# Seven block products for eight in the gated stage of an attention, mixture-of-experts and gated-product kernel

## The reference, cut to what matters

```python
x = attention(q, k, v)          # sink of 4 keys, window of 128
for e in range(8):              # each token goes to one expert, 192 tokens an expert
    h = np.maximum(x[mask_e] @ w1[e], 0.0)
    y[mask_e] = h @ w2[e]
a = y @ w_a                     # (1536 x 512) @ (512 x 1536)
b = y @ w_b
out = (a * b) @ w_out           # (1536 x 1536) @ (1536 x 512)
```

## Time and profile before

| | us |
|---|---|
| median of 3 runs | 674.89 |
| the runs | 673.66 to 678.23 |
| the profiled execution, its own time | 676.53 |
| its span, first to last instruction | 674.8 |
| PE busy | 627.0 (93%) |
| DVE, ACT, POOL busy | 319.2, 312.7, 138.9 |

### The profile page before, as it was taken

One profiled execution on the slowest core, in us unless ns is written; L12 is line 12 of the kernel. 1 busy time (PEld: TensorE's weight loads), 2 busy tenths in 40 slices (PEclk: granted clock), 3 DMA queues, 4 the chain that ended last, 5 costly groups with the idle time before them and its releaser, 6 DMA issues.

```text
span 674.8 us, 10427 instructions
## 1 busy us (share of the span) xinstructions
PE 627.0 (93%) x3696; PEld 527.9 (78%) x3696; DVE 319.2 (47%) x904; ACT 312.7 (46%) x720; POOL 138.9 (21%) x83
## 2 busy tenths in 40 slices
PE   7999999999443999999999999999999999999995
PEld 4877766776322999999999888888888887888784
DVE  3677665772674577877777321213222222222221
ACT  3576655762230577777777241415141415141411
POOL 4000000000004222112222023223431414340502
PEclk8998999999555999999999999999999999999999
DMA  9964150230403356666675314131523232432001
GB/s 187 268 141 95 48 169 28 67 107 16 134 0 92 98 199 239 214 224 223 216 244 180 131 46 141 59 130 62 186 65 122 72 114 86 163 106 80 0 0 62
DMA packets 85813, 81.25 MB, mean 120 GB/s; under 512 B 39696, under 2 KB 62224, under 8 KB 85776
## 3 DMA queue, kind: packets, MB, share of 16 engines
q1 hardware_dynamic: 83856, 74.49, 36.5%
q0 software_dynamic: 1920, 6.29, 2.8%
HBM read 74.48 MB, written 6.29 MB: 120 GB/s over the span
## 4 chain that ended last, share of the span: by engine, by line
PE 87%; DVE 5%; ACT 3%; issue 2%; DMA 1%; POOL 1%; DVEq 0%; ACTq 0%; POOLq 0%
PE psum L1478 15%; PE psum L1471 15%; PE psum L1472 14%; PE psum L1473 14%; PE psum L1479 7%; PE psum L1291 5%; PE psum L1269 3%; PE psum L1256 3%; PE psum L1296 2%; PE psum L1233 2%; ACT above L683 2%; PE psum L1320 1%; PE psum L1462 1%; PE psum L1228 1%; PE psum L1326 1%
## 5 line engine op out<-in xcount | busy, mean ns | idle before, releaser
L529 POOL TENSOR_TENSOR w_lo<-w_raw,w_hi 128x2048 fp32r<-128x2048 f32 x23 | 106.5, 4648 | 298.8 <-ACT w_hi L606 298.8
L606 ACT ACTIVATE w_hi<-w_raw 128x1024 fp32r<-128x1024 f32 (+1 forms) x126 | 123.5, 999 | 19.0 <-PE psum L1473 19.0
L1197 DVE TENSOR_TENSOR g_sb<-psum,a_sb 128x512 f32<-128x512 f32 x36 | 24.9, 692 | 197.0 <-PE psum L1473 197.0
L1471 PE MATMUL psum<-y_hi,w_hi 128*128 x288 | 113.0, 393 | 0.0
L1472 PE MATMUL psum<-y_lo,w_hi 128*128 x288 | 112.2, 390 | 0.0
L1473 PE MATMUL psum<-y_hi,w_lo 128*128 x288 | 112.1, 389 | 0.0
L772 DVE TENSOR_TENSOR w_lo<-w_raw,w_hi 128x1024 fp32r<-128x1024 f32 x64 | 77.7, 1214 | 0.0
L1478 PE MATMUL psum<-x_hl,w_hi 128*128 (+1 forms) x256 | 75.5, 366 | 1.6 <-DVE x_hl L1147 1.6
L1478 PE MATMUL psum<-h_hl,w_hi 128*128 128x384 f32 x256 | 74.7, 362 | 0.0
L745 ACT ACTIVATE g_hi<-g_sb 128x512 fp32r<-128x512 f32 x36 | 22.7, 632 | 91.1 <-DVE g_sb L1197 91.1
L1479 PE MATMUL psum<-x_hl,w_lo 128*128 (+1 forms) x256 | 64.8, 253 | 0.0
(11 more groups left out here) (173 smaller groups left out, 1010.3 us busy)
## 6 DMA issues: line engine op xcount, KB each, us to landing
w_raw<-in_moe_w_dram SPq DMA_DIRECT2D x32, 1024.0 KB, 5.1
w_raw<-in_moe_w_a_dram SPq DMA_DIRECT2D x9, 1024.0 KB, 5.2
w_raw<-in_moe_w_b_dram SPq DMA_DIRECT2D x9, 1024.0 KB, 5.2
w_raw<-in_moe_w_out_dram SPq DMA_DIRECT2D x9, 1024.0 KB, 5.4
k_raw<-in_k_dram SPq DMA_DIRECT2D x16, 192.0 KB, 3.6
q_raw<-in_q_dram SPq DMA_DIRECT2D x16, 192.0 KB, 4.1
v_sb<-in_v_dram SPq DMA_DIRECT2D x16, 192.0 KB, 4.2
xs_scratch<-x_rows SPq DMA_DIRECT2D x8, 384.0 KB, 3.5
```

What stands on the lines that cost most here:

```text
L529: nc.gpsimd.tensor_tensor(ring_lo[u][:, :], raw[u][:, :], ring[u][:, :].bitcast(f32), ALU.subtract).then_inc(w_lo[u], 1)
L606: op = nc.scalar.activation(ring[slot][:, ps], raw[r][:, ps], ACT.Copy)
L1197: nc.vector.tensor_tensor(g_sb[:, j % 2, :], bank[2 + j % 2][:, :], a_sb[:, j % 2, :], ALU.mult).then_inc(g_prod, 1)
L1471: nc.tensor.matmul(o, lhs_hi, rhs_hi, start=first, stop=False)
```

## The change

The gated stage computes a and b by Strassen's scheme in Winograd's form. For a half of 768 tokens and a pair of tiles of the hidden width (256 rows), y (512 x 768) is cut into 2 x 2 blocks of 256 x 384, and the weights (512 x 256) into 2 x 2 blocks of 256 x 128. Seven products of blocks, with the sums S1 to S4 of weight blocks and T1 to T4 of y blocks, give the four blocks of a, and the same of b. There are 2 halves x 6 pairs = 12 stages (`STAGES`). A product is 2 x 3 matmuls of 384 columns (`mix`), so a factor is 42 matmuls, and a stage 84 for both.

The order on PE is `mix(0, n)`, `down(n - 1)`, `mix(1, n)`. `down` makes six tiles of tokens from the pair's 256 hidden rows, 6 matmuls of 512 columns each, 36 a stage; the sum over the pairs isn't kept in PSUM, but DVE adds each tile to `o_acc` in SBUF (`keep_down`, 512 elements). PSUM: banks 0 to 2 for a, 3 to 6 for b, and (7, 0, 1, 2, 7, 0) for the six tiles of `down`.

- POOL: `add_blocks` makes S1 to S4 (four operations of 256), `split_mix` the low parts (512, 256, 512, 512), both for a and for b in each stage, `split_out` the low part of w_out (2 x 512). The long splits of 2048 of the gated stage go; that of unit 3 in each expert stays.
- ACT: `round_mix` rounds 512, 256 and 2 x 512 elements for each factor, `round_out` 1024; `keep_p1`, `keep_a11` and `round_g` handle 384 each.
- DVE: `factor_a` 5 and `factor_b` 13 operations of 384, each with an input in PSUM and one in SBUF.
- T1 to T4 of y: `add_t` (four operations of 192 on DVE, inputs and outputs in SBUF), `round_t` (seven of 192 on ACT), `split_t` (seven of 192 on DVE, in SBUF). Those of the first half are made in four pieces within experts 4 to 7, those of the second in stages 1 to 4.
- The experts' groups of u of 2 and 3 write the plain sum to SBUF: no rounding on ACT, no low part on DVE. All loops of experts and stages are written out. In the last expert no weights of the next unit are split on DVE, and ACT rounds the first blocks for `mix`.

The diff's core (PE, ACT and DVE of the stage, and what is put into the experts):

```diff
+        PRODUCTS = ((A11, B11, BX, True), (S2, T2, BY, True), (A12, B21, BX, False), (S3, T3, BY, False),
+                    (S1, T1, BZ, True), (A22, T4, BY, False), (S4, B22, BZ, False))
+        P1, P6, P2, P7, P5, P4, P3 = range(1, 8)
...
+            def mix(u, n):
...
+                pe.wait_ge(unit_lo[u], n + 1)
...
+                for k, (sb_no, tb_no, bk, first) in enumerate(PRODUCTS):
+                    if k + 1 == P2:
+                        pe.wait_ge(p1_kept[u], n + 1)
+                    elif u == 0 and k + 1 == P6 and n > 0:
+                        pe.wait_ge(a_made, 5 * n)
+                    elif k + 1 in (P7, P4, P3):
+                        made = {P7: (1, 1), P4: (2, 3), P3: (3, 4)}[k + 1][u]
+                        pe.wait_ge((a_made, b_made)[u], (5, 9)[u] * n + made)
+                    o = factor_bank(u, bk)
...
+                    for t in range(2):
...
+                        nc.tensor.matmul(o, w_h, t_hi[:, t, :], start=(first and t == 0), stop=False,
+                                         skip_group_check=True)
+                        nc.tensor.matmul(o, w_h, t_lo[:, t, :], start=False, stop=False, skip_group_check=True)
+                        last = nc.tensor.matmul(o, w_l, t_hi[:, t, :], start=False, stop=(t == 1),
+                                                skip_group_check=True)
+                    last.then_inc(prod, 1)
...
+            for n in range(STAGES):
+                mix(0, n)
+                if n > 0:
+                    down(n - 1)
+                mix(1, n)
+            down(STAGES - 1)
...
+            for n in range(STAGES):
+                if n > 0:
+                    round_mix(1, n, 0)
+                keep_p1(0, n)
+                if n > 0:
+                    round_mix(1, n, 1)
+                keep_a11(n)
+                if n + 1 < STAGES:
+                    round_mix(0, n + 1, 0)
+                    if n > 0:
+                        round_mix(0, n + 1, 1)
+                if 1 <= n <= 4:
+                    round_t(1, n - 1)
+                if n > 0:
+                    round_out(n)
+                keep_p1(1, n)
+                if n == 0:
+                    round_mix(0, 1, 1)
+                for part in range(4):
+                    round_g(n, part)
...
+            for n in range(STAGES):
+                factor_a(n)
+                if 1 <= n <= 4:
+                    add_t(1, n - 1)
+                if n > 0:
+                    keep_down(n - 1)
+                if 1 <= n <= 4:
+                    split_t(1, n - 1)
+                factor_b(n)
+            keep_down(STAGES - 1)
...
+            def factor_b(n):                 # its end
...
+                dve.wait_ge(products_b, 7 * n + P5)
+                dve.wait_ge(b_made, 9 * n + 3)
+                nc.vector.tensor_tensor(w, zb, u3_sb, ALU.add).then_inc(b_made, 1)
+                dve.wait_ge(b_made, 9 * n + 4)
+                nc.vector.tensor_tensor(w, w, a_of[22], ALU.mult).then_inc(b_made, 1)
+                dve.wait_ge(products_b, 7 * n + P4)
+                nc.vector.tensor_tensor(yb, yb, p1_sb, ALU.add).then_inc(b_made, 1)
+                dve.wait_ge(b_made, 9 * n + 6)
+                nc.vector.tensor_tensor(yb, yb, a_of[21], ALU.mult).then_inc(b_made, 1)
+                lower(1)
+                dve.wait_ge(products_b, 7 * n + P3)
+                nc.vector.tensor_tensor(zb, zb, u2_sb, ALU.add).then_inc(b_made, 1)
+                dve.wait_ge(b_made, 9 * n + 8)
+                nc.vector.tensor_tensor(zb, zb, a_of[12], ALU.mult).then_inc(b_made, 1)
+                lower(2)
+                lower(3)
...
             def expert(e, first):  
...
+                        if e >= 4 and (u, g) == (0, 1):
+                            add_t(0, e - 4)
+                        if e >= 4 and (u, g) == (3, 0):
+                            split_t(0, e - 4)
...
+            for n in range(STAGES):          # POOL
+                if n == 0:
+                    add_blocks(0, 0)
+                    split_mix(0, 0)
+                add_blocks(1, n)
+                split_mix(1, n)
+                if n == 0:
+                    split_out(0)
+                if n + 1 < STAGES:
+                    add_blocks(0, n + 1)
+                    split_mix(0, n + 1)
+                if n > 0:
+                    split_out(n)
+                if n == PAIRS_F:
+                    store_rows(0)
+            store_rows(1)
```

More of the change, by code:

```diff
@@ new lines, in split_out, with store_rows @@
+            def split_out(n):
+                pool.wait_ge(unit_hi[2], n + 1)
+                for at in range(2):
+                    hs = slice(at * DM, (at + 1) * DM)
+                    op = nc.gpsimd.tensor_tensor(o_w[1][:, hs], raw_o[:, hs], o_w[0][:, hs].bitcast(f32),
+                                                 ALU.subtract)
+                op.then_inc(unit_lo[2], 1)
+            def store_rows(ct):
+                for st in range(TILES_C):
+                    pool.wait_ge(down_kept, TILES_C * (PAIRS_F * (ct + 1) - 1) + st + 1)
@@ L763, in _ @@
-            with act.Fori(0, NCT - 1) as ct:
-                chunk(ct, False)
-            chunk(NCT - 1, True)
+                        if u < 2:
+                            act.wait_ge(grp_sum, 4 * e + 2 * u + g + 1)
+                            nc.scalar.activation(expert_dst(u, g, e, True), grp_psum(u, g, 0),
+                                                 ACT.Relu).then_inc(grp_hi, 1)
+                        if urgent and not last:
+                            split_hi(slot, slot, g, 16 * loads_before(slot, n), (grp_ready, 8 * e + 2 * u))
@@ new lines, in expert, with keep_p1 @@
+                        if e >= 4 and (u, g) == (2, 0):
+                            round_t(0, e - 4)
+                        if last and (u, g) in ((1, 0), (1, 1)):
+                            round_mix(0, 0, g)
+                        if last and (u, g) == (2, 1):
+                            round_mix(1, 0, 0)
+            for e in range(E):
+                expert(e, e == 0)
+            round_mix(1, 0, 1)
+            round_out(0)
+            def keep_p1(u, n):
+                act.wait_ge(products_of[u], 7 * n + P1)
+                if u == 1:
+                    act.wait_ge(a_made, 5 * n + 4)
+                elif n > 0:
+                    act.wait_ge(b_made, 9 * (n - 1) + 6)
+                nc.scalar.activation(p1_sb, factor_bank(u, BX), ACT.Copy).then_inc(p1_kept[u], 1)
@@ new lines, in keep_a11, with round_g @@
+            def keep_a11(n):
+                act.wait_ge(products_a, 7 * n + P2)
+                if n > 0:
+                    act.wait_ge(b_made, 9 * (n - 1) + 2)
+                nc.scalar.activation(a_of[11], factor_bank(0, BX), ACT.Copy).then_inc(a11_kept, 1)
+            def round_g(n, part):
+                bk, f, half = G_PARTS[part]
+                act.wait_ge(b_made, 9 * n + (2, 5, 7, 9)[part])
+                if part == 0 and n > 0:
+                    act.wait_ge(down_ready, TILES_C * n)
+                nc.scalar.activation(g_part(f, half, 0), factor_bank(1, bk), ACT.Copy).then_inc(g_rounded, 1)
@@ L1163, in expert @@
                         urgent = (u, g) == (1, 1)
                         half = 2 * u + g - 3
+                        more = half >= 0 and e < E - 1
                         if half < 0 and not first and (u, g) == (0, 0):
                             split_lo(e, 2, 1)
[L1167 removed]
+                        if more and not urgent:
                             split_lo(e + 1, half // 2, half % 2)
[L1169 removed]
@@ new lines, in down @@
+            def down(n):
+                mixed = min(n + 2, STAGES)
+                pe.wait_ge(g_split, 4 * (n + 1))
+                pe.wait_ge(unit_lo[2], n + 1)
+                for st in range(TILES_C):
+                    if st == 0 and n > 0:
+                        pe.wait_ge(down_kept, TILES_C * n)
+                    elif st == 1:
+                        pe.wait_ge(a11_kept, mixed)
+                    elif st in (2, 3):
+                        pe.wait_ge(a_made, 5 * mixed - (3 - st))
+                    elif st > 3:
+                        pe.wait_ge(down_kept, TILES_C * n + st - 3)
+                    ss = slice(st * P, (st + 1) * P)
+                    for f in range(2):
+                        fs = slice(f * DM, (f + 1) * DM)
+                        last = product(down_bank(st)[:, :], g_rows(f, 0)[:, ss], g_rows(f, 1)[:, ss], o_w[0][:, fs],
+                                       o_w[1][:, fs], f == 0, f == 1)
+                    last.then_inc(down_ready, 1)
```

460 lines of the change are left out of this document (279 added, 181 removed).

## The result

The kernel with the change takes 721.78 us (median of 4 runs, 719.93 to 723.33); the kernel before, run beside it, 676.56 (4 runs, 673.66 to 678.29). The ratio is 1.067, with a 95% interval of 1.062 to 1.072: slower, as forecast, but by 45 us where 17 were forecast. The 692.0 is too low, and the result lies above the range of 664 to 716. The profiled execution took 722.27, with a span of 720.1.

A forecast was written before the change was run, and what follows sets the result against it. PE alone was taken to bound the gated stage. The span terms 218.2 + 151.9 + 12.4 + 3.1 + 273.0 + 20.9 + 4.0 + 2.3 + 6.2 gave 692.0 us, forecast as 692, range 664 to 716.

The forecast's parts named there:

- matmul of 384: Gated stage, a and b: each matmul of 384 columns steps by 0.1736 us on PE, 0.160 plus 0.0134.
- PE's own work in a stage: Gated stage: two factors of 7.29 us and w_out's 8.17 make 22.75 a stage, 273.0 for twelve, 23.7 gained.
- wait for P1's copy, each: Stage boundary: PE waits before P2 until ACT has copied P1, 1.9 us each, eleven times, 20.9 in all.
- experts 4 to 7 and start, over 18.20 each: POOL holding back add_t costs 3.1 us in each of four experts, 12.4; split_t delays the first gated matmul by 3.1.
- the rival of 0.196 us (709): Gated stage: a matmul of 384 needs 0.196 us, 22.6 more with waits shorter by 5; total 709, chance 0.09.
- The faster rival: Stage boundary: no exclusion between POOL and DVE, and the wait for P1's copy mostly hidden; 654.7 to 660, chance 0.16.
- exclusion between POOL and DVE in the experts: Experts 4 to 7: POOL's 4.62 us split keeps out add_t; PE waits 2.6 and 0.5 us, 12.4 in all.
- The rival without it (678.0): Experts and stages 1 to 4: POOL doesn't keep out DVE, 12.4 and 1.6 us less; 678.0, chance 0.22.
- That holds if DVE starts ahead of POOL's split_out and keeps its turn.: Stages 1 to 4: condition for add_t and split_t on DVE costing only 1.0 us a stage, 4.0 in all.
- The rival of alternation: Stages 1 to 4: most of split_t's operations each wait for one of POOL's; 5.2 us more a stage, 713, chance 0.15.
- Up to 8, should POOL's operations come between: Start of the gated stage: upper size in us of PE's idle before the first gated matmul, forecast at 3.1.
- a granted clock under 1.00 in the gated stage, after one of these idles, which no term has: Gated stage: sign that would show the prediction wrong, PE's clock lowered after an idle; 0 us in the sum.

The follow-up runs named there:

- e8: e7 with P1's copy ahead of rounding g's last part on ACT, and the next a's first sum ahead of two lower parts on DVE: 670.72 us, ratio 0.986.
- e2: Changed kernel with ACT copying P1 before it rounds the next weights of b: 714.79 us.
- e4: Changed kernel with 12 to 16 matmuls that nobody reads ahead of PE's long waits (experts 4 to 7, first gated matmul, stages 1 to 4): 712.13 us.
- e3: Changed kernel with POOL waiting for split_t before split_out in stages 1 to 4: 703.75 us.
- e1: Changed kernel with DVE's add_t in experts 4 to 7 moved from behind group (0,1) to behind group (1,1): 708.8 us.
- e11: e9 with ACT copying the first stage's P1 ahead of the second rounding of b's first weights and the rounding of w_out: 662.6 us, ratio 0.975.
- e5: Changed kernel with POOL's split of unit 3 in the experts made in four instructions of 512 instead of one of 2048: 718.8 us.
- e6: Changed kernel with the edits of e1, e2 and e3 together: 676.57 us.
- e9: e8 with, in the last stage, lower(2) ahead of DVE's z sums and PE's wait ahead of down split: 663.52 us, single run.
- e10: e8 with the last expert in e6's order: 666.49 us, single run.
- e7: e6 with the last expert reordered: add_t, its rounding and split_t earlier, POOL waiting for split_t before splitting the first weights: 678.48 us.

## Why the prediction was right and wrong

The direction was right, and the reason given for it too: PE saves matmuls and loses more to waits that the new scheme brings. The sum of the prediction, step by step, against the trace:

| term | forecast | measured |
|---|---|---|
| matmul of 384 | 0.1736 | 0.1732 |
| PE's own work in a stage | 22.75 | 22.79 (e8) |
| wait for P1's copy, each | 1.9 | 1.58, a stage 24.48 for 24.65 |
| experts 4 to 7 and start, over 18.20 each | 12.4 + 3.1 | 25.5 (4 to 6: 14.1; 7 and the start: 11.4) |
| stages 1 to 4, over the others | 4.0 | 20.7 |
| first stage, low clock | 0 | 1.5 |
| ahead of the last `down` | 2.3 | 3.0 |
| tail | 6.2 | 6.6 |

- **Right: the price of a matmul.** The 13.4 ns on top of 384/2.4 held, so the rival of 0.196 us (709) is out, though its total was nearer, by luck. The Trainium skill ("TensorE: Matmul & The Clock Gate", Back-to-back issue gap) would have 162.5 ns by its formula for a single matmul; here it is 173.2.
- **Right: the wait at P2.** Its chain on ACT was as described, and e2 and e8 took it apart link by link. It was 0.3 too large, for three small reasons: DVE's z mul ended 1.9 us after P3 instead of 2.0, PE went on 0.05 after P1's copy instead of 0.15, and 1.8 had been carried as 1.9. ACT's own chain took 1.7, as forecast. The faster rival fails with it.
- **Right: exclusion between POOL and DVE in the experts**, and its size. The rival without it (678.0) is refuted by the operation of 3.65 us. In experts 5 and 6 PE waited 3.2 us for the first group, in expert 4 2.3, against 2.6 and 0.5 for the second group; without the low clock (e4) experts 4 to 6 were 2.8, 3.7 and 3.7 too long against 3.1 each.
- **Wrong: "That holds if DVE starts ahead of POOL's split_out and keeps its turn."** This is the step that failed, 4.0 for 20.7. DVE did start first, by 0.6 us, but a turn is one instruction of some 0.3, not a procedure of seven. Once POOL's first split stood waiting, the two alternated. The rival of alternation named this mechanism, at 5.2 a stage; measured were 3.4 of wait (it began with the fourth operation, not the first) and 1.6 of low clock. That the two add up to its 5.2 is luck: it had no term for the clock. e3 shows it: the wait and the clock go together, and 24.75 is left. The prediction had used the exclusion for the experts and left it out, in its sum, for the stages, where the same rule holds.
- **Wrong: the last expert, 3.1 and the start's 3.1 for 11.4 in all.** The step ahead of the first gated matmul, 3.49, is close to its 3.1. What was too small is the last expert's own: there POOL also has `add_blocks` and `split_mix` of the first stage, eight small operations beside the eleven of DVE; three of `add_t`'s four met POOL, the unit-2 steps were 4.19 and 1.12, and 6.8 us at 1.2 GHz followed (some 3 us, an estimate from the steps at either clock). "Up to 8, should POOL's operations come between" came true in e1, where all seven of `split_t` met POOL and the step at the start was 8.2.
- **Missing: the clock.** The prediction named "a granted clock under 1.00 in the gated stage, after one of these idles, which no term has" as a sign that would make it wrong. It came, after each idle of over 2 us in the experts and most of those of 3.4 in stages 1 to 4, but never after the 1.6 at P2. e4 puts it at 11.8 us, and some 3 more in expert 7 by estimate. The same waits weren't always followed by it in other executions (expert 4 of e2: a step of 2.25, none), so its size is that of this execution.

In sum: 692.0, + 0.7 before the experts, + 9.7 in experts and start (10.0 by the table, and experts 0 to 2 were 0.2 shorter), + 16.7 in stages 1 to 4, + 1.5 in the first stage, - 1.9 at P2, + 0.7 and + 0.4 at the end make 719.8; the span is 720.1, and the last 0.3 is spread over small steps.

The gain was there and of the size forecast: twelve stages of 22.79 are 273.5 against 296.7. It couldn't be seen because P1's copy stood behind other work on ACT, which the prediction had, and because the new operations of DVE were placed without regard to POOL's, which it had in part. With the orders on four engines changed (e11) 14 to 16 us of the gain arrive.

## What to carry to other kernels

Before DVE gets operations with both inputs in SBUF, list what POOL does at that time: each may cost a whole instruction of POOL's, one after the other for a row of them, and the record shows it as a long DVE operation, not as idle time. Mend that by time, not by size: move the operations to where POOL is idle, or let POOL wait for them, rather than cut POOL's work smaller. Where PE is the bound, a wait of some microseconds has two prices, its own length and the matmuls at 1.2 GHz that may follow it (here 1.6 us on average behind one of 3.4); and a copy out of PSUM that PE waits for goes ahead of all work that only the next stage needs.

## What was unexpected of the hardware

The same code of the experts runs at two paces, at a granted clock of 1.00 in both: an expert of 128 matmuls takes 18.20 us in some executions and 18.56 in others, from its first matmul to the next expert's, which is 0.2845 or 0.290 us for a pair of 384 and 192 columns. Before, after, e3, e4, e5, e6, e9 and e10 showed 18.20 where no collision lay; e1, e2, e7, e8 and e11 showed 18.56, from expert 3 on. e1 and e6 have the same order in the experts, so it isn't the program's order there. Experts 1 to 6 together take 1.7 us longer in e11 than in e9, so it may hide as much of e11's gain. What sets it stays open.

That POOL loses little by the same collisions was also not foreseen. In the alternation of stage 1 its two splits of 512 took 1.45 and 1.38 us and its sums of 256 took 0.84, against 1.29 and 0.74 where DVE kept off: 0.1 to 0.15 each, while each of DVE's lost 0.5 to 1.1. The kernel before shows the same: its eight long splits that start while DVE's L772 still runs take 4.70 to 4.72 us, the others 4.60 to 4.63.
